# Eighty products into an unused PSUM bank while VectorE inverts the second pair's blocks

## What is computed

```python
k_n = k / (norm(k) + 1e-6)
for t in range(S):                       # attention, state is D x D for each head
    y[t] = q[t] @ state
    state = state + beta[t] * outer(k_n[t], v[t] - k_n[t] @ state)
h = maximum(x @ w_in, 0); x1 = (h * h) @ w_out          # dense layer
e = argmax(x1 @ w_gate); out = gate * (maximum(x1 @ w1[e], 0) @ w2[e])   # experts
```

## Time and profile before

| | |
|---|---|
| Runs | 980.75, 982.99, 983.39 us; median 982.99 us |
| Profiled execution | 980.26 us, of which the span of the profile is 978.5 us |
| PE busy | 898.4 us (92% of the span), 10408 instructions |
| DVE busy | 465.6 us (48%) |
| ACT busy | 426.4 us (44%) |
| POOL busy | 193.9 us (20%) |
| Mean granted clock of TensorE | 0.977 of full |

### The profile page before, as it was taken

One profiled execution on the slowest core, in us unless ns is written; L12 is line 12 of the kernel. 1 busy time (PEld: TensorE's weight loads), 2 busy tenths in 40 slices (PEclk: granted clock), 3 DMA queues, 4 the chain that ended last, 5 costly groups with the idle time before them and its releaser, 6 DMA issues.

```text
span 978.5 us, 26066 instructions
## 1 busy us (share of the span) xinstructions
PE 898.4 (92%) x10408; PEld 770.5 (79%) x10409; DVE 465.6 (48%) x971; ACT 426.4 (44%) x745; POOL 193.9 (20%) x146
## 2 busy tenths in 40 slices
PE   3171999999999999999999999997999999999998
PEld 3161788788877888788888888876989898989997
DVE  6989779646744675467432124243222323223221
ACT  4051746653566347634643465651333333333332
POOL 3000000000000000000000003335686623376311
PEclk9995899999999999999999999998999999999999
DMA  7005559933764377336742795706576743362100
GB/s 317 1 11 219 196 180 313 378 135 117 273 227 133 129 250 275 132 124 225 228 142 99 226 353 205 279 1 224 174 274 225 271 161 137 129 259 74 64 20 9
DMA packets 36893, 175.85 MB, mean 180 GB/s; under 512 B 4574, under 2 KB 7812, under 8 KB 30914
## 3 DMA queue, kind: packets, MB, share of 16 engines
q1 hardware_dynamic: 30242, 144.83, 41.6%
q0 software_dynamic: 6560, 29.70, 8.6%
HBM read 147.76 MB, written 28.12 MB: 180 GB/s over the span
## 4 chain that ended last, share of the span: by engine, by line
PE 85%; DVE 9%; issue 2%; ACT 2%; DMA 1%; POOL 1%; DVEq 0%; POOLq 0%; ACTq 0%
PE HP L1112 7%; PE ACC L1125 7%; PE HP L1113 6%; PE HP L1114 6%; PE ACC L1127 6%; PE ACC L1126 6%; PE HP L1484 4%; PE ACC L1516 4%; PE ACC L1515 4%; PE ACC L1517 4%; PE HP L1486 4%; PE HP L1485 4%; PE P L1016 3%; PE P L1495 2%; PE P L1043 2%
## 5 line engine op out<-in xcount | busy, mean ns | idle before, releaser
L355 POOL TENSOR_TENSOR we_l<-raw_e,we_h 128x768 fp32r<-128x768 f32 x16 | 29.5, 1849 | 611.0 <-ACT we_h L481 611.0
L726 DVE TENSOR_TENSOR h_l<-h,h_h 128x512 fp32r<-128x512 f32 x96 | 66.4, 692 | 174.2 <-ACT h_h L455 174.1
L447 ACT ACTIVATE relu<-HP 128x512 f32<-128x512 f32 x96 | 57.4, 598 | 199.7 <-PE HP L1114 199.2
L1112 PE MATMUL HP<-x_h,ring 128*128 128x512 f32 x288 | 119.8, 416 | 0.6 <-DVE x_l L719 0.6
L1125 PE MATMUL ACC<-h_h,ring 128*128 128x512 f32 x288 | 116.9, 406 | 1.4 <-DVE h_l L726 1.4
L1113 PE MATMUL HP<-x_h,ring 128*128 128x512 f32 x288 | 113.9, 396 | 0.1
L1114 PE MATMUL HP<-x_l,ring 128*128 128x512 f32 x288 | 113.7, 395 | 0.0
L1127 PE MATMUL ACC<-h_l,ring 128*128 128x512 f32 x288 | 113.0, 392 | 0.0
L1126 PE MATMUL ACC<-h_h,ring 128*128 128x512 f32 x288 | 112.9, 392 | 0.0
L1326 POOL TENSOR_TENSOR we_l<-raw_e,we_h 128x1536 fp32r<-128x1536 f32 (+2 forms) x24 | 84.1, 3523 | 20.5 <-DMA we_h<-in_w 19.9
L1428 DVE TENSOR_TENSOR hT_l<-P,hT_h 128x512 fp32r<-128x512 f32 x60 | 38.7, 686 | 96.0 <-ACT hT_h L1377 96.0
(11 more groups left out here) (206 smaller groups left out, 1693.6 us busy)
## 6 DMA issues: line engine op xcount, KB each, us to landing
ring<-w_scratch SPq DMA_DIRECT2D x80, 768.0 KB, 4.8
raw_e<-in_w SPq DMA_DIRECT2D x16, 1536.0 KB, 6.8
w_scratch<-ring SPq DMA_DIRECT2D x16, 768.0 KB, 5.0
we_h<-in_w POOLq DMA_DIRECT2D x6, 1536.0 KB, 9.3
kT<-in_kT SPq DMA_DIRECT2D x6, 1024.0 KB, 9.0
kk<-in_k SPq DMA_DIRECT2D x6, 1024.0 KB, 8.2
qT<-in_qT SPq DMA_DIRECT2D x6, 1024.0 KB, 9.6
we_h<-in_w POOLq DMA_DIRECT2D x6, 1024.0 KB, 6.2
```

Source lines behind the costliest of these rows:

```text
L1112: pe.matmul(HP[n % 2][:, :], win_h[:, cols], x_h[:, k, :], start=k == 0, stop=False)
```

## The change

PE's list gets 80 products between `update_state(0, 1)` and `below_blocks(1)`, in four groups. Each multiplies the first weights in `ring` by themselves, 128 rows by 384 columns, into the bank `ACC[1]`, where nothing reads them. The first 20 follow a wait for the fourth masked scores (`mt_done`) and for the first rounded weights (`w_hi`); the other groups (20, 16 and 24) wait for DVE's steps 14, 20 and 26 of the second pair's substitution.

```diff
+        def stay_awake_early(n, bank):
+
+            pe.wait_ge(w_hi, 1)
+            for _ in range(n):
+                pe.matmul(bank[:, 0:DM], ring[:, 0, 0, 0:128], ring[:, 0, 0, :], start=True, stop=True)
+
         def lists():
 
...
         solve(0, 1)
         outputs_of_chunk(0, 1, HP)
         update_state(0, 1)
+        pe.wait_ge(mt_done, 4)
+        stay_awake_early(20, ACC[1])
+        for step, n in ((14, 20), (20, 16), (26, 24)):
+            pe.wait_ge(row_add, NROW + step)
+            stay_awake_early(n, ACC[1])
         below_blocks(1)
         beside_blocks(1)
         pe.wait_ge(ident_done, 2)
```

## The result

The changed kernel takes 992.11 us in the median of five runs (991.19 to 996.30), the kernel before 982.99 (980.75 to 983.63). The ratio is 1.0097, with a 95% interval of 1.0075 to 1.0118. The profiled execution, at 996.3 us, is the slowest of the five, so its trace shows more than the median difference.

A forecast was written before the change was run, and what follows sets the result against it. PE, busy 92% of 978.5 us, was taken as the bound, with its half clock after the 22.8 us wait as the cost. A gain between 0.5 and 0.9, taken as 0.7 us, off the 982.99 median gave 982.3 us, range 978.6 to 985.0.

The forecast's parts named there:

- the sum's first line: On PE, 80 products, 80 weight loads and five waits are added; nothing is removed or moved.
- the 0.7 us: Earlier start of keys_on_state(1, 0), the middle between 0.5 and 0.9 us, carried to the kernel's end.
- The cover of the products: Products on PE from 71.8: 13.6 us at full clock inside the 22.8 us wait before below_blocks(1), 1.4 us spare.
- the gap of 4.1 us: PE idle between the first and second product groups, 75.2 to 79.3; clock expected to fall there in many executions.
- The clock falls again over the 32x32 products: Before up(0, 0) the clock falls again; its nine products at 0.43 us last 3.8 us.
- the rule of the Trainium skill: Only long idle gaps between bursts drop the clock; small products, as busy time, would hold it before up(0, 0).
- Rival one: Clock stays full from 94.5; keys_on_state(1, 0) starts at 102.8, gaining 2.2 us, 980.8 for the median; chance 0.20.
- its two steps: up(0, 0) starts 0.9 us earlier, at about 100.5; keys_on_state(1, 0) starts 0.5 to 0.9 us earlier, middle 0.7.
- Rival three: Last product group at half clock delays below_blocks(1): 2.2 us slower, 4.0 if groups two and three are slow; chance 0.05.

The follow-up runs named there:

- 23 (twice): The changed kernel with 23 calls of 32x32 products ahead of the first group, 256 instructions added in all; 0.9991 and 0.9988 of the kernel before.
- 55 calls: The changed kernel with 55 calls of 32x32 products ahead of the first group, 384 instructions added in all; 0.9996 of the kernel before.
- edges at 220: The changed kernel with 14 or 78 calls of 32x32 products ahead, block edges 220 instructions past a whole block; 1.0029 and 1.0043 of the kernel before.

## Why the prediction was wrong

The forecast was 0.7 us faster, 978.6 to 985.0, with 0.05 for slower by over 0.3%. The step that failed is the sum's first line: "It adds 80 products with 384 columns and 80 weight loads on PE, and five waits; it removes and moves nothing". It moves something: every instruction behind it, against the edges of the blocks in which they arrive. (The number of waits was off too: the trace counts four more semaphore instructions, not five.) That term stood at nothing and is worth 7 to 8 us at this number of instructions (1.0071 with the products left out). With it went "After 105 the chain runs [...] without a point fixed in time near by, so I carry the 0.7 us to the end".

- **The cover of the products** was nearly right: 13.6 us were forecast at full clock, and the rows add up to 16.7 us, in part because two stretches fell at half; they end 1.1 us before `below_blocks(1)`, where 1.4 were forecast. The clock's fall near the gap of 4.1 us came: the granted clock was at half for 3.4 us from 80.1, and it was full again for the last group. DVE's steps did not grow with PE busy beside them: steps 7 to 30 take 18.45 us against 18.41, and the transpose behind them 2.12 against 2.02.
- **The clock falls again over the 32x32 products**: right in the changed kernel, against the rule of the Trainium skill (TensorE: Matmul & The Clock Gate, section "Why this matters for your kernels") that was weighed. The products of `up(0, 0)` stand 0.43 apart here, and in the traces of the kernels with 23 (twice) and 55 calls the clock is at half again between 98 and 100 us. Rival one did occur in one trace, that of the kernel with 46 products of 8 columns, where the last large product ends at 96.4: `up(0, 0)` is 0.23 apart from its first product, and `keys_on_state(1, 0)` waits for `copy_N`, as its terms said. There the clock held through 5.4 us of 32x32 products and short idle times, so these alone do not always bring it down.
- **The 0.7 us** could be seen in the time only with the edges put back: 0.9 and 1.2 us there, with intervals that reach 1.0002 and 1.0000. The traces show its two steps, counted from the start of `below_blocks(1)`. `up(0, 0)` starts after 6.20 to 6.26 us in eight traces with the large products and after 6.66 in a ninth (the one with the last product at 96.4 left out), against 6.89 to 6.91 without them: 0.65 us in most, where 0.9 was forecast, because the first product starts 0.26 us after the weights are there. `keys_on_state(1, 0)` starts after 10.16 to 10.36 us with them and 10.41 to 11.04 without, a median difference of 0.4 us against the 0.7. So the mechanism holds at both steps and is somewhat smaller than forecast; that it lasts to the end of the kernel is not shown.
- **Rival three** ended on the right side by the wrong mechanism: the last group was not late.
- **What the trace of before had shown**: the one pause of 1.66 us in the middle of `beside_blocks`, put down to "issue", and the instruction queue's packets of 16 KB on the page. Both stood in what I had read, but I took into account only the waits up to 110 us and did not ask what an "issue" pause inside a row of equal products is, which was the one place where the changed number of instructions could enter.

What ends a pause is shown: the landing of the block's packet, 1.20 to 1.58 us before. Why that packet comes late at some edges and in time at others with products just as dense stays open. For the 74 pauses it starts between 2.4 us before the pause and 1.0 us after the pause has begun, and the length of a pause differs between kernels at the same edge (1.24, 1.65 and 1.82 us in the Gram products). So the place of the edges is shown as the cause of the 7 to 8 us, not the rule by which one of them hurts.

## What to carry to other kernels

An inserted instruction has a cost that no term for its work contains: it moves all later code of its engine against the blocks of 256 instructions. Before a change on PE is judged, put it beside a control with the same number of instructions and no work, or pad it to a whole block; and look in the waits for "issue" inside a row of equal instructions, whose number in the engine's list tells whether it stands at an edge, and for the packet of the instruction queue that landed just before its end. Differences below 1% between two versions of an unrolled kernel with many small products may be the edges and not the idea.

## Not expected of the hardware

- PE paused up to 3.4 us at a block edge (in `beside_blocks` at 192 us, edges at 220), although the 128 products of that row take 2.2 us.
- The pauses are only part of the lag. Between `up(0, 0)` and `up(5, 15)` it grows by 14.5 us in the profiled execution, of which 8 are the added pauses. From 108 to 650 us the clock is at half for 17.0 us in the changed kernel and for 6.8 in the kernel before, which is where I put most of the rest; no run separates the two.
- A product of 8 columns with its own weight load cost 0.11 us at full clock and 0.21 at half (32 in 3.5 us, 97 in 20.5), which is not far from one of 384 columns (0.17 at full clock), while 82 products of 32x32 took 1.51 us.
